# Two feed-forward stages behind a delta-rule attention: sorted rows scattered to DRAM, against rows kept in token order and gathered through a token list

## The chip, the cores and the metric

The kernel runs on one core of a Trainium2 chip. The metric is the time of the whole program on the device, in microseconds (us). Engines: TensorE (PE) multiplies matrices, VectorE (DVE), ScalarE (ACT) and GpSimd (POOL) work element by element, SyncE (SP) only issues transfers. ACT and POOL issue transfers too.

## What is computed

Four things follow one another; N = 3072 tokens (4 batches of 768), model width 384, hidden width 1024.

```python
for t in range(768):                       # delta-rule attention, 4 x 8 heads of width 48
    y[t] = q[t] @ state
    state += beta[t] * outer(k[t], v[t] - state.T @ k[t])      # k normalised
x = ((x @ w1) * (x @ w2)) @ w3 @ w_out     # dense part, for every token
e = argmax(x @ w_gate + bias[modality])    # one of 8 experts per token
gate = softmax(...)[e]
out[token] = gate * (relu(x @ w1[e]) @ w2[e])
```

The gate's weights are drawn large, so that the tokens fall on few experts: in the profiled execution three experts are loaded and 26 tiles of 128 tokens are computed.

## The kernel before

**First part, to about 652 us.** The tokens go in 24 units of 128 (6 groups of 4, one unit of each batch per group). Each engine has its own program, written out by hand turn by turn: in turn u, unit u is begun and unit u-1 ended, and six places `at` = 0..5 in a turn take one piece each of the dense part of an earlier group (`piece_of`: 24 pieces per group). The dense part of group c is: split of x into two roundings (`split_x`: ACT at L686 makes the upper one, DVE at L941 the rest), 16 products up (`up`, PE at L1427), 8 halves of products down (`down`, PE at L1445), which leave the 384 outputs and 8 logits of each row in `rows` (`take_row`, ACT at L703). `split_x(c)` stands in ACT's and DVE's programs one piece ahead of the group's first piece, behind the last `take_row` of the group before. ACT's `take_whole_t` (L642), which PE's `whole_x` (L1310) needs, stands ahead of that piece.

**Routing of a group**, one group later (DVE `choose`, `count`, `weigh`, `places`; PE `ranks`): the expert of each token, its gate, and its place, which is expert x 3200 plus its rank among the tokens of that expert. POOL's `scatter` (L563) then writes the four sets of 128 rows to `sorted_rows` in DRAM, each row to its place, with the token's number and gate in two more columns. ACT's `take_row` of the next group waits for that.

**Between the parts, about 669 to 712 us.** The last group is routed, PE counts the tokens of each expert, and DVE builds small tables by a chain of some 30 operations (L1120 to L1164): `fill_at`, where each expert's rows end; the order of the experts that have tokens (`ranks_ready`, at L1143); and for each tile its first row in `sorted_rows` and its expert (`table_ready`, at L1164). SP and ACT each write four blocks of 128 rows of padding behind the experts' rows (`fill_after`, L343 and L344), SP then loads the experts' weights (L492, 1.5 MB each for w1 and w2, with the first w2 held back until the first two x tiles have landed), ACT waits for all scatters and fills and loads the x tiles (`load_x`, L783 and L784). Weights are split like x (ACT L790, DVE L1180).

**Second part, the tiles.** The order on each engine for tile n is:

- PE: transposes of the hidden values of n (L1583), up product of n+1 (L1552), transposes of x of n+2 (L1532), down product of n (L1566).
- ACT: load of x of n+2, then the upper halves of the hidden values, perhaps half of a split of weights, hidden values and x of later tiles, the rest of the split.
- DVE: the same with the lower halves; last, when PE has ended the down product of n, `ys` = result x gate (L1215).
- POOL: waits for `ys` of n and writes it with an indirect DMA to the tokens' rows in `out` (L594). The token numbers are a column of the x tile. Padding rows have a number out of bounds and are left out.

The x buffers go round in four (`TURN`), so a load of x may be up to four tiles old. 24 tiles always run; further ones run under a condition (`tiles_that_may_be`), where POOL waits for each store to land (`stored_tile`).

Of the kernel before, what the change touches and what calls it, by code (L numbers as in the profile page):

```python
# [39 lines left out]
ROW = WX + 2  # L40
GATE, TOKEN = WX, WX + 1
CAP = N + P
# [18 lines left out]
def constants():  # L61
# [13 lines left out]
    token = ((u % B)[None, :] * S + (u // B)[None, :] * P + p[:, None]).astype(np.int32)  # L75
    fill = np.zeros((P, ROW), np.int32)
    fill[:, TOKEN] = NO_TOKEN
    small = np.concatenate([
        np.arange(E) - E,
        np.arange(E) * CAP,  # L80
        np.arange(N // P) * P,
        np.repeat(np.arange(TABLE), E),
        np.arange(TABLE) * P,
    ]).astype(np.float32)
    small = np.ascontiguousarray(np.broadcast_to(small, (P, small.size)))
    return {"planes": planes, "planes64": small_planes, "masks": masks, "token": token, "fill": fill, "small": small}
# [4 lines left out]
M_STARTS = M_PLACE + E  # L91
# [5 lines left out]
def program(nc, a, out):  # L97
    sorted_rows = nc.dram_tensor("sorted_rows", [(E + 1) * CAP, ROW], F32, kind="Internal").ap()
# [18 lines left out]
    with top:  # L117
# [9 lines left out]

        rows = sbuf(top, "rows", [P, B, ROW])
        rows_i = rows[:, :, :].bitcast(I32)
        token = sbuf(top, "token_sb", [P, UNITS], I32)  # L130
# [6 lines left out]
        place = sbuf(top, "place", [P, B], U32)  # L137
# [49 lines left out]
        hid = sbuf(late, "hid", [P, FF])  # L187
        raw = sbuf(late, "raw", [P, SLOTS * WE])
        xs = sbuf(late, "xs", [P, TURN, ROW])
        ys = sbuf(late, "ys", [P, TURN, DM])  # L190
        fill = sbuf(late, "fill_sb", [P, ROW], I32)
        fill_at = sbuf(late, "fill_at", [P, E], I32)
        ntile = sbuf(late, "ntile", [P, 4, E])
# [3 lines left out]
        table = sbuf(late, "table", [P, 4, TABLE + 1], I32)  # L197
        numbers = sbuf(late, "numbers", [P, M_END - M_STARTS])
# [7 lines left out]
        def plane64(k, n):  # L206
# [10 lines left out]
            hot_ready rank_done place_ready row_ready scattered dve_step count_done  # L217
            ranks_ready table_ready fill_ready filled expert_w1_in expert_w2_in upper_w1
            upper_w2 lower_w1 lower_w2 x_done xs_upper x_taken hid_done hid0_ready
# [119 lines left out]
        def fill_after(eng, experts_of):  # L339

            eng.wait_ge(q["fill_ready"], 1)
            for e in experts_of:
                row = eng.value_load(fill_at[0:1, e:e + 1], min_val=0, max_val=E * CAP - P)  # L343
                eng.dma_start(sorted_rows[bass.ds(row, P), :], fill[:, :].bitcast(F32)  # L344
                              ).then_inc(q["filled"], 16)
# [1300 lines left out]
```

## Time and profile before

| | before |
|---|---|
| median of 3 runs | 974.9 us (974.3 to 976.1) |
| the profiled execution: its own time | 973.82 us |
| its span, first to last instruction | 971.9 us |
| PE busy, matmul | 888.7 us (91%) |
| DVE / ACT / POOL busy | 490.3 / 343.2 / 274.4 us |
| mean granted TensorE clock | 0.965 of 2.4 GHz |

The profile is of one execution, and durations below come from it. Its time is 1.9 us more than its span, which lies around the instructions, and 1.1 us under the median of the three runs. A busy share is over the whole span, so it hides that the kernel has two dense parts with a gap between them.

### The profile page before, as it was taken

How to read it: one execution, taken by the hardware profiler on the slowest of the kernel's cores; microseconds unless marked ns; L12 is line 12 of the kernel's file. 1: busy time of each engine (PE TensorE's matmuls, PEld its weight loads, DVE VectorE, ACT ScalarE, POOL GpSimd, SP SyncE). 2: the span in 40 equal slices, each digit the busy share in tenths (PEclk: the TensorE clock that was granted, in tenths of full speed). 3: DMA queues.
4: the chain of work that ended last, by engine and by line, in shares of the span. 5: the costliest groups of instructions: out<-in, count | busy, mean ns of one | idle time of the engine just before them, and what ended most of it. 6: DMA issues, size and time to landing. Idle time of an engine off the chain costs nothing.

```text
span 971.9 us, 29550 instructions
## 1 busy us (share of the span) xinstructions
PE 888.7 (91%) x11972; PEld 741.6 (76%) x11973; DVE 490.3 (50%) x891; ACT 343.2 (35%) x628; POOL 274.4 (28%) x296
## 2 busy tenths in 40 slices
PE   5999989999999999899989999996379999999996
PEld 4766657788778877787778778785269899999985
DVE  2567666665755576557654752233265333333332
ACT  1344444444544453345424532220243222222221
POOL 5345544443454344434434210011000111101010
PEclk9999989999999999999989999998679999999998
DMA  7424311111121111111111010101931111111110
GB/s 247 129 84 140 84 38 37 38 38 38 37 72 38 38 38 54 54 38 38 44 52 33 17 45 10 33 33 56 326 143 43 42 42 41 39 46 44 41 41 21
DMA packets 46570, 60.13 MB, mean 62 GB/s; under 512 B 9192, under 2 KB 39160, under 8 KB 45552
## 3 DMA queue, kind: packets, MB, share of 16 engines
q1 hardware_dynamic: 38640, 42.35, 14.5%
q0 software_dynamic: 3200, 9.56, 2.6%
q10 hardware_dynamic: 4608, 6.46, 2.3%
q8 instruction: 93, 1.52, 0.6%
q14 instruction: 29, 0.24, 0.1%
HBM read 42.26 MB, written 11.77 MB: 56 GB/s over the span
## 4 chain that ended last, share of the span: by engine, by line
PE 80%; DVE 5%; POOL 5%; issue 3%; ACT 3%; another core or an unknown queue 1%; DMA 1%; SPq 1%; ACTq 0%; DVEq 0%; POOLq 0%
PE banks L1427 19%; PE banks L1552 12%; PE banks L1445 11%; PE banks L1566 11%; PE banks L1288 4%; PE banks L1397 3%; PE banks L1355 3%; PE banks L1583 2%; PE banks L1365 2%; PE banks L1248 2%; PE banks L1377 2%; POOL nm L543 1%; PE banks L1344 1%; POOL inv L547 1%
## 5 line engine op out<-in xcount | busy, mean ns | idle before, releaser
L1427 PE MATMUL banks<-xr,w12r 128*128 128x512 f32 x864 | 227.9, 412 | 7.6 <-DVE xr L941 7.5
L1427 PEld LDWEIGHTS banks<-xr,w12r 128*128 128x128 f32 x864 | 161.0, 194 | 45.5 <-issue 9.5
L1552 PE MATMUL banks<-experts,kept 128*128 x486 | 124.5, 411 | 11.0 <-DVE experts L1180 8.5
L1552 PEld LDWEIGHTS banks<-experts,kept 128*128 128x128 f32 x486 | 92.6, 195 | 32.4 <-issue 11.7
L1566 PE MATMUL banks<-experts,kept 128*128 x624 | 114.8, 340 | 0.0
L1445 PE MATMUL banks<-kept,hr 128*128 128x392 f32 x576 | 112.2, 347 | 0.0
L1566 PEld LDWEIGHTS banks<-experts,kept 128*128 128x128 f32 x624 | 107.1, 188 | 0.0
L1445 PEld LDWEIGHTS banks<-kept,hr 128*128 128x128 f32 x576 | 100.9, 188 | 2.0
L594 POOL DMA_INDIRECT out<-ys,xs x26 | 25.6, 984 | 259.7 <-DVE ys L1215 259.7
L531 POOL TENSOR_TENSOR kb<-keys,beta_sb 128x384 f32<-128x384 f32 x24 | 29.1, 1213 | 244.4 <-PE banks L1387 244.4
L874 DVE TENSOR_TENSOR picked<-inv,masks_sb 128x512 f16<-128x512 f16 x96 | 47.0, 489 | 77.0 <-ACT inv L630 76.0
L630 ACT ACTIVATE inv<-banks 128x512 f16<-128x512 f32 x96 | 57.2, 596 | 79.0 <-PE banks L1288 63.1
L636 ACT ACTIVATE inv<-banks 128x512 f16<-128x512 f32 x96 | 56.9, 593 | 51.0 <-PE banks L1291 45.0
L881 DVE STREAM_TRANSPOSE corr<-picked 128x512 f16<-128x512 f16 x96 | 68.3, 711 | 3.3
L828 ACT ACTIVATE kept<-banks 128x512 fp32r<-128x512 f32 x52 | 28.3, 596 | 104.4 <-PE banks L1583 104.4
L1288 PE MATMUL banks<-inv,corr 64*64 64x128 f16 x1152 | 47.5, 224 | 11.1 <-DVE corr L881 10.4
L563 POOL DMA_INDIRECT sorted_rows<-rows,place x24 | 23.4, 974 | 114.2 <-DVE place L1041 108.2
L947 DVE TENSOR_TENSOR asb<-asb,banks 128x512 f32<-128x512 f32 x48 | 32.9, 685 | 39.8 <-PE banks L1427 39.8
L1215 DVE TENSOR_SCALAR ys<-banks,xs 128x384 f32<-128x384 f32 x26 | 16.0, 617 | 71.4 <-PE banks L1566 71.4
L1397 PE MATMUL banks<-wo_x,w3T 128*128 128x392 f32 x128 | 51.5, 529 | 0.0
L1171 DVE TENSOR_SCALAR hid<-banks 128x512 f32<-128x512 f32 x27 | 18.6, 691 | 63.6 <-PE banks L1552 63.6
L804 ACT ACTIVATE hid<-banks 128x512 f32<-128x512 f32 x27 | 16.1, 598 | 92.5 <-PE banks L1552 92.5
(144 smaller groups left out, 1318.7 us busy)
## 6 DMA issues: line engine op xcount, KB each, us to landing
raw<-in_moe_w SPq DMA_DIRECT2D x6, 1536.0 KB, 7.3
kq<-in_qT SPq DMA_DIRECT2D x24, 256.0 KB, 2.7
xs<-sorted_rows ACTq DMA_DIRECT2D x28, 197.0 KB, 2.4
kraw<-in_k SPq DMA_DIRECT2D x24, 192.0 KB, 2.4
vals<-in_v SPq DMA_DIRECT2D x48, 96.0 KB, 2.5
w3T<-in_w3T SPq DMA_DIRECT2D x8, 512.0 KB, 4.3
w<-in_w SPq DMA_DIRECT2D x8, 384.0 KB, 4.2
xT<-yT SPq DMA_DIRECT2D x48, 64.0 KB, 2.1
```

The source lines that it names most:

```text
L630: nc.scalar.activation(inv[:, u % 2, 1].rearrange("p (k g) t -> p k (g t)", k=2), all_pairs(1), ACT.Copy).then_inc(right_taken[level], 1)
L636: nc.scalar.activation(inv[:, u % 2, 0].rearrange("p (k g) t -> p k (g t)", k=2), all_pairs(0), ACT.Copy).then_inc(x_taken[level], 1)
L874: nc.vector.tensor_tensor(picked[:], inv[:, u % 2, 1], masks[:, level - 1:level, :].to_broadcast([P, H, R]), ALU.mult).then_inc(masked[lev ...
L881: nc.vector.transpose(corr[:, u % 2, level % 2].rearrange("p g t -> p (g t)"), picked[:].rearrange("p g t -> p (g t)")).then_inc(part_read ...
L947: nc.vector.tensor_tensor(asb[:, j % 2], asb[:, j % 2], psum[:, UP + 1, :], ALU.mult).then_inc(q["h_made"], 1)
L1288: last = mm(pairs_of(g)[rows_of(x)], part, inv[rows_of(x), u % 2, :, g, :], start=True, stop=True)
L1355: last = mm(told_of(o)[rows_of(x), j, :], xfin[rows_of(x), u % 2, o * HH + j, :], rest[rows_of(x), o * HH + j, :], start=True, stop=True)
L1397: last = mm(psum[:, UP + i % 2, 0:WX], w3T[:, i % W_SLOTS, k, :], wo_x[:, k, :], start=(k == 0), stop=(k == FT - 1))
L1427: last = mm(psum[:, UP + w, :], w12r[:, p, w, k, j * P:(j + 1) * P], xr[:, r, k, :], start=(k == 0 and p == r), stop=(k == KT - 1 and p == 1))
L1445: last = mm(psum[:, UP + t % 2, 0:WX], hr[:, p, j, t * P:(t + 1) * P], w34r[:, r, j, :], start=(j == 0 and p == r), stop=(j == FT - 1 and ...
L1552: last = mm(psum[:, f, :], xsr[:, w, p, k, :], experts[:, bass.ds(slot * (2 * WE) + at, FF // 2)], start=(k == 0 and p == r), stop=(k == K ...
L1566: last = mm(psum[:, 4 + w, 0:DM], hTr[:, p, k, :], experts[:, bass.ds(slot * (2 * WE) + at, DM)], start=(k == 0 and p == r), stop=(k == FT ...
```

## The change

Rows go to DRAM in token order, by plain transfers on SP's queue. The row has 385 columns: the gate takes the place of the first logit. POOL's scatters, the padding rows and the fills on SP and ACT are gone. `place` is now expert x 3072 plus rank, taken apart into a lane (0..127) and a column (0..191). In the gap of buffers after the attention, POOL builds for each unit one-hot matrices of lanes, times a token number (`list_lane`, 128 columns), and of columns (`list_column`, 192 columns), in f16; for the last group DVE builds the lanes. PE multiplies them, 24 products summed in one bank, which gives for each expert tile a column of token numbers. DVE makes two indices of them by five operations: one to gather with, one to store with. In the tile loop ACT loads nothing; POOL reads the tile's column number, copies the column of indices to `index_now` and gathers x of n+2 by an indirect DMA, then waits for `ys` of n and stores it, as before. ACT's `split_x` of the groups 1 to 5 stands two pieces ahead of the group instead of one. The wait for the first two x tiles moves from the first expert's w2 to the second expert's w1.

```diff
@@ SP
+                        keep_rows(piece[0] - 1)
+            def keep_rows(c):
+                sp.wait_ge(q["row_ready"], c + 1)
+                sp.dma_start(kept_rows.rearrange("(b c p) n -> c p b n", b=B, c=C)[c], rows[:, :, 0:ROW]
+                             ).then_inc(q["rows_kept"], 16)
-            fill_after(sp, range(0, E, 2))
-                        if k == 0 and name == "w2":
+                        if k == 1 and name == "w1":
                             for w in range(2):
                                 sp.wait_ge(x_in[w], 16)
@@ POOL
-            def scatter(c):
-                for t in range(B):
-                    nc.gpsimd.indirect_dma_start(
-                        sorted_rows[:, :], bass.IndirectOffsetOnAxis(ap=place[:, t:t + 1], axis=0),
-                        rows[:, t, :], None).then_inc(q["scattered"], 16)
+            def list_lane(t):
+                nc.gpsimd.tensor_scalar(lane_is[:, t, :], small[:, M_LANE:M_LANE + P], lane[:, t:t + 1],
+                                        token[:, t:t + 1], ALU.is_equal, ALU.mult
+                                        ).then_inc(q["lane_listed"], 1)
+            def list_column(t):
+                nc.gpsimd.tensor_scalar(column_is[:, t, :], slots[:], column[:, t:t + 1], None, ALU.is_equal
+                                        ).then_inc(q["column_listed"], 1)
+            def gather(n, r):
+                at = pool.value_load(table[0:1, 0, bass.ds(n, 1)], min_val=0, max_val=NO_SLOT)
+                nc.gpsimd.tensor_copy(index_now[:, r, :], index[:, bass.ds(at, 1), :].rearrange("p o k -> p (o k)")
+                                      ).then_inc(q["index_taken"], 1)
+                pool.wait_ge(q["index_taken"], n + 1)
+                alone(pool)
+                nc.gpsimd.indirect_dma_start(
+                    xs[:, r, :], None, kept_rows[:, :],
+                    bass.IndirectOffsetOnAxis(ap=index_now[:, r, 0:1], axis=0)).then_inc(x_in[r], 16)
+            pool.wait_ge(q["table_ready"], 1)
+            pool.wait_ge(q["index_ready"], 1)
+            pool.wait_ge(q["rows_kept"], 16 * C)
+            gather(0, 0)
+            gather(1, 1)
             def tile(i, r):
-                pool.wait_ge(q["ys_ready"], i * TURN + r + 1)
+                n = i * TURN + r
+                ahead = (r + 2) % TURN
+                since(pool, stored[ahead], 16 * (i + (r + 2) // TURN))
+                gather(n + 2, ahead)
+                pool.wait_ge(q["ys_ready"], n + 1)
                 alone(pool)
                 nc.gpsimd.indirect_dma_start(
-                    out[:, :], bass.IndirectOffsetOnAxis(
-                        ap=xs[:, r, TOKEN:TOKEN + 1].bitcast(U32), axis=0),
+                    out[:, :], bass.IndirectOffsetOnAxis(ap=index_now[:, r, 1:2], axis=0),
                     ys[:, r, :], None, bounds_check=N - 1, oob_is_err=False).then_inc(stored[r], 16)
@@ ACT
-                for c in group_begun(u, at, 1):
-                    split_x(c)
+                for ahead in (1, 2):
+                    for c in group_begun(u, at, ahead):
+                        if (c > 0) == (ahead == 2):
+                            split_x(c)
-            fill_after(act, range(1, E, 2))
-                since(act, stored[ahead], 16 * (i + (r + 2) // TURN))
-                load_x(n + 2, ahead)
@@ DVE
+                link(v.tensor_reduce(place[:, now], key, AX.X, ALU.add))
+                link(v.tensor_scalar(column[:, now], place[:, now], 0.5 - P / 2, ROUNDS_TO_P, ALU.add, ALU.add))
+                link(v.tensor_scalar(column[:, now], column[:, now], -ROUNDS_TO_P, None, ALU.add))
+                v.tensor_tensor(lane[:, now], place[:, now], column[:, now], ALU.subtract
+            for t in range(UNITS - B, UNITS):
+                v.tensor_scalar(lane_is[:, t, :], small[:, M_LANE:M_LANE + P], lane[:, t:t + 1],
+                                token[:, t:t + 1], ALU.is_equal, ALU.mult).then_inc(q["last_lane_listed"], 1)
+            dve.wait_ge(q["slots_found"], 1)
+            link(v.tensor_scalar(late_at[:], numbered, 0.0, float(N + 1), ALU.is_lt, ALU.mult))
+            link(v.tensor_tensor(found[:], numbered, late_at[:], ALU.add))
+            v.tensor_scalar(index[:, 0:NO_SLOT, 0], found[:], -1.0, 0.0, ALU.add, ALU.max)
+            link(v.tensor_scalar(late_at[:], found[:], 0.0, float(NO_TOKEN), ALU.is_equal, ALU.mult))
+            v.scalar_tensor_tensor(index[:, 0:NO_SLOT, 1], found[:], -1.0, late_at[:], ALU.add, ALU.add
+                                   ).then_inc(q["index_ready"], 1)
@@ PE
+                    last = mm(psum[:, 5, 0:NO_SLOT], lane_is[:, t, :], column_is[:, t, :],
+                              start=(t == 0), stop=(t == UNITS - 1))
+            place_tokens(range(UNITS - B))
             ranks(C - 1)
             mm(psum[:, 6, 0:E], planes[:, C_ONE, :], seen[:], start=True, stop=True
                ).then_inc(q["count_done"], 1)
+            place_tokens(range(UNITS - B, UNITS)).then_inc(q["slots_found"], 1)
```

## Rows read from the trace of the kernel before

**Rows 1.** Page, part 4: share of the chain that ended last, by engine.
```profile
PE 80%; DVE 5%; POOL 5%; issue 3%; ACT 3%; another core or an unknown queue 1%; DMA 1%; SPq 1%; ACTq 0%; DVEq 0%; POOLq 0%
```
**Rows 2.** Stretches: length, busy of PE, PEld, DVE, ACT, POOL, clock, DMA, GB/s.
```profile
672.00:691.00 19.00, 1.66 (x7) 1.60 (x8) 8.35 (x43) 0.62 (x1) 3.84 (x4) 0.50 0.74 232
...
724.00:940.00 216.00, 216.00 (x1193) 195.25 (x1192) 80.08 (x119) 52.81 (x95) 22.64 (x23) 1.00 0.12 41
```
**Rows 3.** Chain of work at the first tiles: start, us, what.
```profile
728.01 0.33 PE banks L1532 x3
728.34 4.17 PE banks L1566 x24
```
**Rows 4.** Chain, one tile in the middle.
```profile
742.08 0.87 PE banks L1583 x8
...
747.18 0.33 PE banks L1532 x3
```
**Rows 5.** Timeline of that tile: start, length, what, idle before.
```profile
742.12 0.62 DVE L1215 TENSOR_SCALAR ys<-banks,xs 128x384 f32<-128x384 f32 x1 [2.93 <-PE banks L1566]
...
743.62 0.98 POOL L594 DMA_INDIRECT out<-ys,xs  x1 [5.69 <-DVE ys L1215]
```
**Rows 6.** POOL's prices: transfer to landing; value load (ns); gap between scatters; two operations.
```profile
out<-ys,xs POOLq DMA_INDIRECT x26, 2.5
...
L334 POOLq TENSOR_LOAD <-table x1: 502/502/502, 947.6 to 947.6; - x1
...
POOL sorted_rows L563 <- issue: 5.1, 18, 0.3
...
L543 POOL TENSOR_TENSOR nm<-am,planes_sb 128x256 f16<-128x256 f32 x48 | 37.0, 770 | 12.8 <-DVE am L865 12.8
...
L583 POOL MEMSET keys<- 128x128 f32 x1 | 0.2, 204 | 0.3 <-POOLq L1638 0.3
```
**Rows 7.** L784, the 28 loads of x tiles: issue to landing.
```profile
DMA to landing us min/median/max: 2.1/2.4/8.6
```
**Rows 8.** Timeline of the first tiles, where ACT and DVE also split weights.
```profile
725.83 0.61 DVE L1215 TENSOR_SCALAR ys<-banks,xs 128x384 f32<-128x384 f32 x1
...
728.95 2.77 ACT L790 ACTIVATE experts<-raw  x1
...
732.16 3.36 DVE L1180 TENSOR_TENSOR experts<-raw,experts  x1
```
**Rows 9.** Timeline between the parts.
```profile
672.29 0.64 PE L1455 MATMUL banks<-hot,planes_sb 128*128 128x32 f32 x2 [3.04 <-DVE seen L1018]
...
674.14 0.36 DVE L1120 TENSOR_TENSOR over<-banks,numbers 128x192 f32<-128x192 f32 x1
...
675.71 5.01 SPq L344 DMA_DIRECT2D sorted_rows<-fill_sb  x4
...
677.63 0.17 DVE L1143 CAST table<-ttab 128x8 int32<-128x8 f32 x1
...
681.72 0.24 DVE L1164 TENSOR_SCALAR table<-ttab 128x33 int32<-128x33 f32 x1
```
**Rows 10.** Chain between the parts.
```profile
682.87 7.24 DMA raw<-in_moe_w
...
694.90 6.54 PE banks L1552 x18
```
**Rows 11.** Timeline at a boundary of groups; last, that wait over all groups (total, times, longest).
```profile
231.75 0.60 ACT L642 ACTIVATE inv<-banks 128x512 f16<-128x512 f32 x1 [0.37 <-PE banks L1301]
...
233.98 0.44 PE L1310 MATMUL banks<-inv,corr 64*64 64x64 f16 x16
...
234.48 1.66 ACT L686 ACTIVATE xr<-xT 128x512 fp32r<-128x512 f32 x3
...
236.82 2.29 PE L1427 MATMUL banks<-xr,w12r 128*128 128x512 f32 x9 [1.45 <-DVE xr L941]
...
PE banks L1427 <- DVE xr L941: 7.5, 6, 1.9
```

More of the change, by code:

```diff
@@ L39 @@
 E_SCALE = 1024.0
-ROW = WX + 2
-GATE, TOKEN = WX, WX + 1
-CAP = N + P
+GATE = DM
+ROW = DM + 1
+CAP = N
+HI = CAP // P
+NO_SLOT = E * HI
+ROUNDS_TO_P = float(3 * P << 22)
 TILES = N // P + E - 1
@@ L136, in program @@
         lred = sbuf(top, "lred", [P, 5, B])
[L137 removed]
+        place = sbuf(top, "place", [P, UNITS])
+        lane = sbuf(top, "lane", [P, UNITS])
+        column = sbuf(top, "column", [P, UNITS])
         work = ExitStack()
@@ L438, in turn @@
                     send(u - 2)
+                for at in range(SPLITS):
+                    piece = piece_of(u, at)
+                    if piece and piece[0] and piece[1] == WEIGH:
+                        keep_rows(piece[0] - 1)
[3 more added lines that the diff above has]
+                             ).then_inc(q["rows_kept"], 16)
             load_k(0)
@@ L464, in _ @@
             sp.wait_ge(q["y_taken"], UNITS + 1)
-            sp.dma_start(fill[:], a["fill"]).then_inc(q["b_in"], 16)
+            sp.dma_start(slots[:], a["slots"]).then_inc(q["slots_in"], 16)
             sp.dma_start(numbers[:], a["small"][:, M_STARTS:]).then_inc(q["b_in"], 16)
-            sp.wait_ge(q["b_in"], 80)
-            sp.dma_start(sorted_rows[E * CAP:E * CAP + P, :], fill[:, :].bitcast(F32)
-                         ).then_inc(q["filled"], 16)
-            fill_after(sp, range(0, E, 2))
+            for u in range(UNITS + 2, last_turn() + 1):
+                for at in range(SPLITS):
+                    piece = piece_of(u, at)
+                    if piece and piece[0] and piece[1] == WEIGH:
+                        keep_rows(piece[0] - 1)
+            keep_rows(C - 1)
             sp.wait_ge(q["ranks_ready"], 1)
@@ L573, in turn @@
                     beta_mask(u + 1)
-                for at in range(SPLITS):
-                    piece = piece_of(u - 1, at)
-                    if piece and piece[0] and piece[1] == RANK:
-                        scatter(piece[0] - 1)
                 if live(u + 1):
@@ L585, in _ @@
             pool.wait_ge(q["const_in"], 64)
-            for u in range(-2, last_turn() + 1):
+            for u in range(-2, UNITS + 1):
                 turn(u)
-            scatter(C - 1)
-            def tile(i, r):
-                pool.wait_ge(q["ys_ready"], i * TURN + r + 1)
+            pool.wait_ge(q["y_taken"], UNITS + 1)
+            for b in range(B):
+                pool.wait_ge(sent[b], 64 * C)
+            nc.gpsimd.memset(index[:, NO_SLOT, 0:1], 0)
+            nc.gpsimd.memset(index[:, NO_SLOT, 1:2], NO_TOKEN).then_inc(q["no_slot_set"], 1)
@@ new lines, in _ @@
+            pool.wait_ge(q["b_in"], 64)
+            pool.wait_ge(q["slots_in"], 16)
+            for c in range(C):
+                pool.wait_ge(q["place_ready"], c + 1)
+                for t in range(c * B, c * B + B):
+                    if c < C - 1:
+                        list_lane(t)
+                    list_column(t)
+            def gather(n, r):
[3 more added lines that the diff above has]
+                pool.wait_ge(q["index_taken"], n + 1)
```

101 lines of the change are left out of this document (52 added, 49 removed).

## The prediction

> **What bounds the kernel now.** I read the chain of waits first: PE holds 80% of it [rows 1]. Then the stretches: from 724 to 940 us PE is busy all the time at the full clock, and from 672 to 691 us it does almost nothing, at half clock [rows 2]. So there are two dense parts, where whatever delays PE lengthens the run, and a gap between them, set by a chain through DVE, SP's transfers and ACT. The timeline then shows, in each part, what stands closest to PE's path. The change touches three places: group boundaries in the first part, the gap, and every tile of the second. I take the tiles first, because 25 of them multiply whatever one costs.
>
> **Tiles: where the new load of x stands.** In a tile of the middle PE ends a down product at 742.08, transposes and does the up product, and wants x of the tile after next at 747.18, 5.10 us later [rows 4]. Today ACT asks for that x well ahead, so nobody waits. After the change POOL asks for it, and POOL is in order: the gather for tile n+2 stands behind the store of tile n-1, which stands behind `ys` of n-1, which stands behind PE's down product of n-1. The four buffers don't help, since the request itself is late. The path from there, step by step:
> - `ys` runs 742.12 to 742.74, and the store on POOL 743.62 to 744.60 [rows 5]: both stay.
> - The value load takes 0.50 us on POOL [rows 6], with register work some 0.75 (estimate). It may run under the store (0) or after it (0.75). The sequencer should be free while the engine writes descriptors, so I take 0.2.
> - The copy of 128x2 numbers: POOL's 128x128 memset takes 0.20 [rows 6], so 0 to 0.2; I take 0.1.
> - The gather waits for that copy by semaphore, like the store for `ys`: the store starts 0.88 after `ys` ends [rows 5]. Back to back, without a wait, the gap is 0.3 [rows 6]. I take 0.88, because the wait is there; 0.3 is the low end.
> - Landing: 2.5 us from the start for the indirect store [rows 6], 2.1 at the least for plain loads of x [rows 7]. An indirect load is not in the trace; I take 2.5, ends 2.1 and 2.6.
>
> So x lands at 744.60 + 0.2 + 0.1 + 0.88 + 2.5 = 748.28, which is **1.1 us after PE wants it**, and 5.54 after `ys` ends. The low ends give 747.0, just in time (0); the high ones 749.03 (1.9). The wait can't be made up: PE's down product is behind the transposes of x, `ys` behind that, and the next gather behind `ys`. The loop becomes a ring of DVE, POOL, DMA and PE, and each tile pays.
>
> 26 stores mean 26 tiles [rows 6], and gathers 0 to 27. The first three are asked ahead of any store, so 25 can be late. Four of them are special:
> - x 3: DVE does `ys` of tile 0 late, behind a split of weights, ending 726.44 [rows 8]. x lands at 731.98; PE wants it at 728.01 [rows 3]: 4.0.
> - x 4: ACT's split started 0.94 after the transposes of x 3 and takes 2.77, DVE's then 3.36, `ys` 0.61 [rows 3, 8]. From 731.98 that is 739.7, and x 4 lands at 745.2. PE wants it 0.33 + 4.17 + 5.10 after 731.98, at 741.6: 3.7.
> - x 26: the loop has ended, POOL waits for the last store to land (0.88 + 2.5 after `ys`), does two value loads (1.5), copy, start and landing (3.48): 8.4 against 4.44, so 3.9.
> - x 27: the same with one value load: 3.2.
>
> Sum: 14.8 for the four, and 21 x 1.1 = 23.1 for the others: **+37.9**. With the low ends the four give 10.5 and the others 0; with the high ones 18 and 40.
>
> **Group boundaries.** PE waits 7.5 us in six places for the split of x [rows 11], and at the one shown ACT begins it at 234.48, behind the last `take_row`. One piece earlier it goes ahead of L642 at 231.75 and takes 1.66, so L642 ends at some 234.0 and PE's L1310, which needs it, is at 233.98: no loss beyond 0.1. DVE has the operands 2.7 us earlier, more than the 1.45 that PE waited. The first group keeps its place. 5/6 of 7.5: **-6.2**; ends 0 (if the y values have not landed by then, ACT holds up everything behind) and -7.5.
>
> **Removed from the first part.** POOL's scatters and two small DVE operations per group cost nothing today: POOL sits idle before the keys of each turn, and no chain went through them. SP's `keep_rows` waits for the gates, which are made earlier in the same turn than the y values SP has just waited for: nothing queued behind it is late. If it were, the loads of k and q two turns ahead would cover it. The one-hots of the first 20 units are made by POOL after 615 us, 40 operations of 0.2 to 0.77 us each [rows 6], at most 31 us, before 669. PE's 20 products fit in the 3.04 us in which it waited before 672.29 [rows 9] if each takes up to 0.15 us. If not, each tenth of a microsecond more is 2 us. I count 0.
>
> **The gap.** DVE gains two small operations in `places`, four one-hots (0.25 each, between small operations and the 0.36 of 128x192 [rows 9]) and loses one: +1.3, so the tables are ready at 681.96 + 1.3 = 683.3 [rows 9]. Five operations of 0.4 for the indices follow: 685.3. Then value load, copy and start (0.75 + 0.1 + 0.88): the first gather begins at 687.0. SP loses the fills, which kept it until 680.72 [rows 9]; it then needed 2.15 us to send w1 [rows 10]. Now it starts when the order of the experts is there, at 677.8 + 1.3 = 679.1 [rows 9], w1 goes at 681.3 and lands at 688.5, 1.6 sooner. But w2 of the same expert now goes right behind it, 1.5 MB more, and until some 695 the gather shares the DMA engines with it. Loads of x took 2.4 in the median and 8.6 at most, the latter with weights in flight [rows 7]. Alone the first x lands at 689.5, and then w1 sets the start: 1.6 gained. With 8.6 it lands at 695.6; transposes, ACT and DVE (some 1.8) put the first up product at 697.4 against 694.90 [rows 10], 2.5 lost. I take nearly that end, **+2.0**, since the weights are in flight the whole time.
>
> The Trainium skill (DMA: Bandwidth & Descriptors, Queues, rings and completion order) says that each DMA engine takes turns between queues packet by packet, with some 9 to 17 descriptors in a typical packet. The 8 rows that an engine has of a gather would then be one packet, and pass after one packet of weights; by this the gap would gain the 1.6 and the sum would be 3.6 lower. The 8.6 us row speaks against it.
>
> **Sum.** +37.9 - 6.2 + 2.0 = +33.7 on the profiled 973.8, so 1007.5, and the median lies 1.1 above: **1008.6 us**.
>
> **Rivals.**
> 1. *The gather just makes it* (chance 0.08). With all low ends the steady wait is 0; the four special ones (10.5), the boundaries (-7.5) and the gap (-1.6) leave +1.4: 976. For it: each low end is in a row. Against it: all four have to hold together, and the semaphore latency of 0.88 is seen at each store.
> 2. *Faster* (0.07). Besides rival 1, w2's early arrival lets DVE do `ys` of tiles 0 and 1 without a split of 3.36 us ahead of it, and the special waits shrink from 10.5 to about 4: 4 - 7.5 - 1.6 = -5, 970. It decides at a path from `ys` to landed x of 4.44 us; I get 5.54.
> 3. *The clock falls* (0.05). If gaps in every tile make the chip grant half the clock, as it does in the idle stretch [rows 2], an up product takes 6.54 instead of 4.2 us [rows 10], and a tile some 5 us more: +125, 1130. Against it: the first part has a wait of 1.45 us [rows 11] and runs on.
> The forecast has 0.80. Its own ends are +15 (steady wait 0.5) and +60 (1.9, and nothing gained at the boundaries): 990 to 1035. The range, 980 to 1038, also takes in part of rival 1. About 0.2% is what a measurement of this kernel can tell from no change; that bound and the cases give faster 0.08, same 0.03, slower 0.89.
>
> **What would show it.** Right: PE's L1532 twin waits for the DMA of x about 1.1 us in each of some 21 tiles, and 3 to 4 us in four; a period of some 10.7 us instead of 9.6 (5.10 + 0.33 + 4.17); POOL's idle time before its store shrinks to about 5 us. The waits of L1427 on L941 all but vanish. The first gather takes more than 6 us to land. Wrong: if POOL's gather starts less than 1 us after the store ends, or an indirect load lands in 2 us or less, the steady wait goes and rival 1 or 2 holds; if the gather starts over 2 us behind the store, the time is above 1030.

## The result and the profile after

On the same chip the changed kernel takes 1034.5 us in the median of 4 runs (1031.6 to 1042.7), the kernel before 975.4: ratio 1.062, 95% interval [1.056, 1.068], so **59 us slower**. The forecast was 1008.6 in a range of 980 to 1038.

| | before | after |
|---|---|---|
| the profiled execution: its own time | 973.82 us | 1035.74 us |
| its span | 971.9 us | 1033.9 us |
| PE busy, matmul | 888.7 us (91%) | 911.2 us (88%) |
| DVE / ACT / POOL busy | 490.3 / 343.2 / 274.4 us | 503.3 / 346.0 / 328.4 us |
| mean granted TensorE clock | 0.965 | 0.951 |

The page after, its first part and the chain that ended last. Where nothing but PE held a large share before [rows 1], the transfer of `xs` has 8% of the chain now:

```profile
PE 911.2 (88%) x11996; PEld 756.5 (73%) x11997; DVE 503.3 (49%) x905; ACT 346.0 (33%) x628; POOL 328.4 (32%) x375
...
PE 66%; DMA 9%; issue 8%; DVE 8%; POOL 5%; ACT 2%; POOLq 2%; DVEq 0%; SPq 0%; ACTq 0%
PE banks L1482 19%; PE banks L1637 12%; PE banks L1500 10%; DMA xs<-kept_rows,index_now 8%; PE banks L1343 4%; PE banks L1410 3%; PE banks L1452 2%; PE banks L1303 2%; PE banks L1420 2%; PE banks L1432 2%; DVE ys L1270 2%; PE banks L1603 2%; PE banks L1623 1%; PE banks L1399 1%; DVE xr L981 1%
```

The timeline of one tile in the middle, the twin of [rows 4, 5] (start, length, what, and in brackets the idle time before and what ended it):

```profile
802.33 0.62 DVE L1270 TENSOR_SCALAR ys<-banks,xs 128x384 f32<-128x384 f32 x1 [3.52 <-PE banks L1637]
...
802.72 4.44 PE L1623 MATMUL banks<-experts,kept 128*128 x18
...
803.87 1.02 POOL L645 DMA_INDIRECT out<-ys,index_now  x1 [8.89 <-DVE ys L1270]
804.86 0.23 POOL L621 COPY index_now<-index 128x2 uint32 x1
805.89 0.99 POOL L626 DMA_INDIRECT xs<-kept_rows,index_now  x1 [0.80 <-POOL index_now L621]
...
809.01 0.55 PE L1603 MATMUL banks<-planes_sb,xs 128*128 128x128 f32 x3 [1.85 <-DMA xs<-kept_rows,index_now]
...
809.50 6.01 PE L1637 MATMUL banks<-experts,kept 128*128 x24
```

The ring of the prediction is there: `ys`, store, copy, gather, landing, PE. PE has ended its up product at 807.16 and stands until 809.01. Two things are not as predicted. The gather takes 3.12 us from its start to PE's first transpose (I took 2.5). And the 24 products of the down product behind the wait take 6.01 us, where 13 of the 21 tiles from 3 to 23 show 4.5 in the same view. In the 6 us before PE's transposes the granted clock is 1.00, in the 6 us behind them 0.72, between its two levels, so a part of this product ran at half the clock (length; busy of PE, PEld, DVE, ACT, POOL; clock, DMA, GB/s). The third line has the whole stretch from 724 to 990 us, where before the clock was 1.00 and PE was never idle [rows 2]:

```profile
803.00:809.00 6.00, 4.16 (x18) 3.00 (x16) 1.98 (x3) 1.68 (x3) 2.22 (x3) 1.00 0.20 66
809.00:815.00 6.00, 5.99 (x26) 5.83 (x27) 0.56 (x1) 0.49 (x1) 0.00 (x0) 0.72 0.00 0
...
724.00:990.00 266.00, 228.55 (x1139) 200.61 (x1139) 66.89 (x107) 45.84 (x85) 46.54 (x63) 0.94 0.10 31
```

Of the waits of that stretch (total, times, longest) PE's for x is the one that is new:

```profile
PE banks L1603 <- DMA xs<-kept_rows,index_now: 37.5, 21, 2.2
```

The view of the tile `xs` gives the time from a gather's issue to its landing. The 7.4 is the third gather, issued at 667.37 us beside the experts' weights; nothing waited for it.

```profile
DMA to landing us min/median/max: 3.0/3.2/7.4
```

**Where the time went.** With the starts of `ys` as milestones (tile 0 at 725.83 before and 699.87 after, tile 2 at 742.12 and 730.11, tile 23 at 943.44 and 989.94, tile 25 at 962.61 and 1024.19), the two spans compare like this:

| stretch | before | after | change | predicted |
|---|---|---|---|---|
| start to tables ready | 681.96 | 658.28 | -23.7 | -4.9 |
| tables to the first up product | 12.94 | 10.70 | -2.2 | +0.7 |
| to `ys` of tile 0 | 30.93 | 30.89 | 0 | 0 |
| tiles 1 and 2 | 16.29 | 30.24 | +13.9 | +7.7 |
| tiles 3 to 23 | 201.32 | 259.83 | +58.5 | +23.1 |
| tiles 24 and 25 | 19.17 | 34.25 | +15.1 | +7.1 |
| to the end | 9.29 | 9.71 | +0.4 | 0 |
| sum | | | +62.0 | +33.7 |

The direction is right, and every large term is too small: the tiles lost more than twice what I gave them, and the first part gained 19 us that I did not see at all. These two are what the experiments are about.

### The profile page after: what moved, and what is told of

Same layout as the page of the kernel before. It is cut to its first block, busy times and chain, and to the rows that moved or that the text cites. A ratio compares the mean times of both kernels' runs of the same rounds, so it can differ in the third digit from the quotient of the medians.

```text
span 1033.9 us, 29628 instructions
## 1 busy us (share of the span) xinstructions
PE 911.2 (88%) x11996; PEld 756.5 (73%) x11997; DVE 503.3 (49%) x905; ACT 346.0 (33%) x628; POOL 328.4 (32%) x375
## 4 chain that ended last, share of the span: by engine, by line
PE 66%; DMA 9%; issue 8%; DVE 8%; POOL 5%; ACT 2%; POOLq 2%; DVEq 0%; SPq 0%; ACTq 0%
PE banks L1482 19%; PE banks L1637 12%; PE banks L1500 10%; DMA xs<-kept_rows,index_now 8%; PE banks L1343 4%; PE banks L1410 3%; PE banks L1452 2%; PE banks L1303 2%; PE banks L1420 2%; PE banks L1432 2%; DVE ys L1270 2%; PE banks L1603 2%; PE banks L1623 1%; PE banks L1399 1%; DVE xr L981 1%
## 5 line engine op out<-in xcount | busy, mean ns | idle before, releaser
L1482 PE MATMUL banks<-xr,w12r 128*128 128x512 f32 x864 | 222.4, 404 | 0.7 <-DVE xr L981 0.7
L1482 PEld LDWEIGHTS banks<-xr,w12r 128*128 128x128 f32 x864 | 156.8, 189 | 36.3 <-DVE xr L981 1.1
L1637 PE MATMUL banks<-experts,kept 128*128 x624 | 135.9, 381 | 0.0
L1623 PE MATMUL banks<-experts,kept 128*128 x486 | 124.2, 410 | 8.5 <-DVE experts L1235 8.1
L1637 PEld LDWEIGHTS banks<-experts,kept 128*128 128x128 f32 x624 | 127.9, 219 | 2.9 <-issue 0.7
L1623 PEld LDWEIGHTS banks<-experts,kept 128*128 128x128 f32 x486 | 92.8, 196 | 29.4 <-issue 9.2
L645 POOL DMA_INDIRECT out<-ys,index_now x26 | 26.5, 1020 | 274.9 <-DVE ys L1270 274.9
L1603 PE MATMUL banks<-planes_sb,xs 128*128 128x128 f32 x84 | 17.4, 322 | 71.1 <-DMA xs<-kept_rows,index_now 71.0
L1603 PEld LDWEIGHTS banks<-planes_sb,xs 128*128 128x128 f32 x84 | 9.9, 156 | 82.9 <-DMA xs<-kept_rows,index_now 68.8
```

What stands on the lines that cost most here:

```text
L1482: last = mm(psum[:, UP + w, :], w12r[:, p, w, k, j * P:(j + 1) * P], xr[:, r, k, :], start=(k == 0 and p == r), stop=(k == KT - 1 and p == 1))
L1603: last = nc.tensor.transpose(psum[:, 6 + r % 2, k * P:(k + 1) * P], xs[:, r, k * P:(k + 1) * P], ident)
L1623: last = mm(psum[:, f, :], xsr[:, w, p, k, :], experts[:, bass.ds(slot * (2 * WE) + at, FF // 2)], start=(k == 0 and p == r), stop=(k == K ...
L1637: last = mm(psum[:, 4 + w, 0:DM], hTr[:, p, k, :], experts[:, bass.ds(slot * (2 * WE) + at, DM)], start=(k == 0 and p == r), stop=(k == FT ...
```

## The experiments

Twelve kernels ran, four to a chip. The kernel before does not take the same time on every chip: 956.2 us on chip 6 (e1 to e4), 974.6 on chip 1 (e5 to e8), 974.0 on chip 8 (e9 to e12). So ratios are against the kernel before on the same chip, and the difference itself became a question (e3, e11, e12). The profiled execution of the kernel before belongs with the 974s.

### e1: the gathers asked for one tile earlier

```diff
+            gather(2, 2)
...
-                ahead = (r + 2) % TURN
-                since(pool, stored[ahead], 16 * (i + (r + 2) // TURN))
-                gather(n + 2, ahead)
+                ahead = (r + 3) % TURN
+                since(pool, stored[ahead], 16 * (i + (r + 3) // TURN))
+                gather(n + 3, ahead)
```

> The changed kernel with one edit: POOL gathers x of tile n+3 instead of n+2, into the buffer of tile n-1, once that tile's store has landed. Theory A (the tiles lose because the request for x is late, and the falling clock is only a consequence of PE's waits): POOL asks some 5.3 us after ys, x lands some 8.5 us after ys, PE wants it 14 us after ys, so no wait; the period goes back to 9.6 us, the clock to 1.00, the tile part from 348 to 260 us from the second up product on: time about 947 us, 28 below the kernel before. Rival B (software gathers on POOL slow PE or the transfers whatever their place): waits of 1 us or more per tile stay, time above 975.

Measured: 948.4 us, 0.9914 [0.9895, 0.9933] of the kernel before. The stretch of the tiles:

```profile
724.00:910.00 186.00, 186.00 (x1029) 169.00 (x1029) 61.43 (x98) 40.36 (x78) 42.59 (x58) 1.00 0.13 40
```

PE is busy all the time at the full clock, and `ys` comes every 9.4 to 9.8 us, as before. Tiles 3 to 23 take 201.81 us (201.32 before), and the four special tiles lose no more than 0.2 us. The ring was the whole loss in the tiles. The gather itself is no faster (3.2 us in the median); it is only behind a store one tile older. On this chip this kernel is 0.9% faster than the kernel before.

### e2: the index taken a tile ahead, the gather in its old place

```diff
+            def take_index(n, r):
                 at = pool.value_load(table[0:1, 0, bass.ds(n, 1)], min_val=0, max_val=NO_SLOT)
                 nc.gpsimd.tensor_copy(index_now[:, r, :], ...
                                      ).then_inc(q["index_taken"], 1)
+            def gather(n, r):
...
-                since(pool, stored[ahead], 16 * (i + (r + 2) // TURN))
                 gather(n + 2, ahead)
+                after = (r + 3) % TURN
+                since(pool, stored[after], 16 * (i + (r + 3) // TURN))
+                take_index(n + 3, after)
```

> The changed kernel with one edit: the value load and the copy of the index column for tile n+3 stand ahead of the wait for ys, so that only store and gather stand behind it; the gather stays where it was. Theory A (the steps I listed, in series): the copy (0.23 us) and the part of the 0.80 us start that a wait costs (0.5, since starts back to back are 0.30 apart) leave the ring; the full-clock period goes from 11.7 to 11.0 us, time about 1034 - 25 x 0.7 = 1017, less if the clock holds more often. Rival (the start of an indirect DMA costs 0.8 us by itself whatever precedes it): 0.23 only, about 1028.

Measured: 1004.1 us, 1.0499 [1.0475, 1.0523]. Its timeline at a store, a gather and the transposes that wait for it:

```profile
805.15 1.02 POOL L652 DMA_INDIRECT out<-ys,index_now  x1 [7.30 <-DVE ys L1277]
806.47 1.00 POOL L628 DMA_INDIRECT xs<-kept_rows,index_now  x1 [0.31 <-issue]
...
809.76 0.55 PE L1610 MATMUL banks<-planes_sb,xs 128*128 128x128 f32 x3 [1.14 <-DMA xs<-kept_rows,index_now]
```

The gather follows the store by 0.31 us in place of 1.00, and PE's wait drops from 1.85 to 1.14: the same 0.7 us. Tiles 3 to 23 take 233.6 us (11.1 each). The clock in its tiles is 1.00, with a wait of 1.1 in each tile. So the copy and the semaphore behind it are 0.7 us of the ring. The expectation had 1017 us for these 0.7 in 25 tiles; the time is 13 us below it, and it had allowed for that where the clock holds, as it does here. Of what is left of the ring, the landing is the largest step.

### e3: the scatters put back beside e1

Four groups' rows are written by index where POOL had its scatters; they go to rows of DRAM that nobody reads.

```diff
+            def spare(c):
+                pool.wait_ge(q["place_ready"], c + 1)
+                pool.wait_ge(q["row_ready"], c + 1)
+                alone(pool)
+                for t in range(B):
+                    nc.gpsimd.indirect_dma_start(
+                        spare_rows[:, :], bass.IndirectOffsetOnAxis(ap=spot[:, t:t + 1], axis=0),
+                        rows[:, t, 0:ROW], None).then_inc(q["spared"], 16)
...
+                    since(act, q["spared"], 16 * B * min(c, 4))
...
+                link(v.tensor_copy(spot[:], place[:, now]))
```

The last two lines are ACT's wait for the writes ahead of its next rows, and a small copy on DVE that makes the index.

> e1 with POOL's indirect writes of the rows put back at their old place in POOL's turns for groups 0 to 3, to a tensor nobody reads (plain transfers on SP stay too). Theory C (the first part gained 24 us mostly because these writes are gone: they hold up ACT, DVE and PE for 4 us each time): the tables are ready 16 to 20 us later than in e1, time e1 + 18, ACT waits of 4.3 us from a releaser that the profile can't name come back. Rival D (the gain came from the earlier split of x and from the granted clock): e1 + 1 or less.

Measured: 949.7 us, 0.9926 [0.9905, 0.9947], 1.35 above e1, where the runs of each spread over 1.2 and 2.2 us. The expected 18 us are not there. Nor is the 1.35 in the first part: the last `ys` begins at 936.55 us (936.48 in e1), and the difference is behind it, 11.1 us to the end against 9.8. e11 and e12 have the same longer end, for which no trace shows a reason. On this chip the scatters are nearly free.

### e4: e1 with the split of x back in its place

```diff
-                for ahead in (1, 2):
-                    for c in group_begun(u, at, ahead):
-                        if (c > 0) == (ahead == 2):
-                            split_x(c)
+                for c in group_begun(u, at, 1):
+                    split_x(c)
```

> e1 with ACT's split of x put back to one piece ahead of its group. Theory C: PE waits for the split again, 1.5 to 1.9 us at five boundaries: e1 + 6. Rival D: e1 + 20 or more.

Measured: 955.0 us, 0.9987 [0.9976, 0.9999], **6.6 above e1**. PE's waits in the first part (total, times, longest), e4:

```profile
PE banks L1481 <- DVE xr L980: 7.5, 6, 2.0
```

and the same line in e1:

```profile
PE banks L1483 <- DVE xr L982: 0.5, 1, 0.5
```

The wait of [rows 11] is back, 7.5 in six places, and costs nearly what it says. The term of -6.2 was right. On chip 6, e1 + 6.6 (split) + 1.35 (scatters) = 956.3, and the kernel before takes 956.2 there. That the sum fits so closely is in part luck: the 1.35 is at the end of the program, the kernel before was not traced on this chip, and the rest of the change (lists, tables, gap) is not in the sum.

### e5 and e6: both kernels once more, on another chip

> The kernel before, unchanged, for a profile beside the others. In e1 to e4 it took 956.2 us where the first measurement had 975.4, and e3 showed the scatters at 1.3 us. Theory F (the 4.3 us stalls of all engines in the turns with scatters belong to the place where the program runs, and not to the scatters alone): the profile of a run of 956 us has the scatters at the same places and no such stall, its tables are ready at 663 us instead of 682, and the tile part is 260 us as before. Rival G (the tile part or the gap is what differs): the 19 us are found behind 669 us.

> The changed kernel, unchanged, beside e5, e7 and e8. Theory F: it has no scatters in the first part, so it takes the same 1032 to 1040 us here, and the change costs some 78 us instead of 59 where the kernel before takes 956. Rival G: it gains 19 us as well, 1015.

Neither has an edit. e5 (the kernel before): 974.9 us, 0.9997 [0.9986, 1.0009], the same; one of its ten runs took 1697.6, for which no trace shows a reason. e6 (the changed kernel): 1038.9 us, 1.0649 [1.0627, 1.0671]. A trace of the kernel before at 956 us, which would show what it takes 18 us more for on this chip, is missing. e5's waits from 250 to 640 us have a candidate (total, times, longest):

```profile
ACT inv L630 <- remote: 12.8, 3, 4.3
...
DVE corr L893 <- remote: 9.3, 3, 3.3
...
ACT inv L636 <- remote: 6.7, 1, 6.7
```

"remote" is a wait that no instruction of the profile ends. The waits of ACT and DVE run in part at the same time, so their sum is not the loss. The profile of before had them too: its page shows "another core or an unknown queue 1%" [rows 1]. e6 has none.

### e7: the changed kernel with PE kept busy in the wait

```diff
+                for _ in range(16):
+                    nc.tensor.transpose(psum[:, 6 + r % 2, 384:512], ident, ident)
```

The 16 transposes of a unit matrix stand between the up product and the transposes of x; nothing reads them.

> The changed kernel with one edit: in every tile PE does 16 transposes of the identity (0.11 us each) into free columns between the up product and the transposes of x, where it waits. Theory H (down products of 5.9 us are ones at half the clock, and the clock falls because PE waits some 2 us in each tile): PE has hardly any gap, the clock is 1.00 in the tile part, every down product takes 4.2 to 4.4 us, the period is 11.7 us in all tiles: 1.6 us less in some 9 tiles, about 1020. Rival (the slow down products come from something else, the gather's traffic for one): they stay at 5.9 us, 1034 or more.

Measured: 1022.5 us, 1.049 [1.0464, 1.0516]: **16.4 below e6, with more work**. The stretch in e6:

```profile
724.00:990.00 266.00, 228.41 (x1115) 200.75 (x1114) 66.09 (x106) 45.69 (x84) 46.66 (x63) 0.92 0.10 31
```

and in e7:

```profile
724.00:990.00 266.00, 258.20 (x1520) 230.94 (x1521) 69.44 (x110) 47.87 (x88) 48.86 (x66) 1.00 0.11 33
```

The clock is 1.00 in place of 0.92. The timeline of e7 shows a tile in which the ring is untouched and only the gap is filled:

```profile
800.08 0.62 DVE L1270 TENSOR_SCALAR ys<-banks,xs 128x384 f32<-128x384 f32 x1 [3.51 <-PE banks L1637]
...
804.74 1.91 PE L1659 MATMUL banks<-planes_sb 128*128 128x128 f32 x16
...
806.68 0.55 PE L1603 MATMUL banks<-planes_sb,xs 128*128 128x128 f32 x3
807.14 4.50 PE L1637 MATMUL banks<-experts,kept 128*128 x24
...
811.67 0.62 DVE L1270 TENSOR_SCALAR ys<-banks,xs 128x384 f32<-128x384 f32 x1 [3.33 <-PE banks L1637]
```

x still arrives 6.60 us after `ys` begins, and the down product takes 4.5. Tiles 3 to 23 take 247.3 us, against 264.2 in e6 and 201.3 before. That separates the two parts of e6's loss there: 46.0 from the ring at the full clock (2.2 a tile) and 16.9 from the clock. Eleven of e6's 21 down products there take 5.9 to 6.0 us, 1.5 more than the others, which is the same 16.9 within 0.4. The filling does not help the last two tiles, whose waits are longer (34.7 us against 33.4).

### e8: a plain read in the gather's place

The choice of rows is left out: each tile reads the first 128 rows in DRAM.

```diff
-                nc.gpsimd.indirect_dma_start(
-                    xs[:, r, :], None, kept_rows[:, :],
-                    bass.IndirectOffsetOnAxis(ap=index_now[:, r, 0:1], axis=0)).then_inc(x_in[r], 16)
+                pool.dma_start(xs[:, r, :], kept_rows[0:P, :]).then_inc(x_in[r], 16)
```

> The changed kernel with POOL's gather replaced by a plain read, from POOL's queue too, of the same 128 rows of 385 numbers each time: it leaves out the choice of rows, so the outputs are of other tokens. Theory I (an indirect load takes 3.1 us to land where plain ones take 2.4 because of the rows' own addresses): landing 2.4 to 2.6, period 11.1, waits 0.6 us shorter in 25 tiles, time 1018 or, if the clock holds, 1005. Rival (a load on POOL's queue takes 3.1 us whatever it reads): the same time as e6.

Measured: 1004.8 us, 1.0303 [1.0285, 1.0322], 34 below e6. The view of `xs` in e8:

```profile
DMA to landing us min/median/max: 2.6/2.7/4.7
```

and one of its reads in the timeline:

```profile
810.62 0.56 POOL L626 DMA_DIRECT2D xs<-kept_rows  x1 [0.60 <-POOL index_now L621]
```

The plain read starts 0.60 after the copy (0.80) and lands in 2.7 us (3.2): 0.7 us less per tile, and with that the clock mostly holds (0.99 from 724 to 960). It is e2's saving by another way, and e2's time within 0.7 us, though on another chip.

### e9: the second weight matrix held back again, beside e1

```diff
-                        if k == 1 and name == "w1":
+                        if k == 0 and name == "w2":
```

> e10 with SP's wait for the first two row tiles put ahead of the first expert's second weight matrix, as the kernel before had it (it now stands ahead of the second expert's first matrix). Theory, that the second matrix's transfer is what makes the first gather land 4.6 us after its start in the changed kernel, where those in the loop take 3.1: the first gather lands about 1.5 us sooner, the first up product begins 1 to 1.5 us sooner, and the time is 1 to 1.5 us under e10's unless the second matrix's own split then comes late. Rival, that a first gather is slow for another cause, or that the chain into the first up product runs through other work: no change within 0.5 us, or slower by up to 2 us for the later matrix.

Measured: 948.3 us, 0.9727 [0.9702, 0.9753]; e10, its reference, 947.5. No gain. The first gather and the first transposes in e9:

```profile
662.53 1.19 POOL L626 DMA_INDIRECT xs<-kept_rows,index_now  x1 [0.92 <-POOL index_now L621]
...
666.49 0.87 PE L1604 MATMUL banks<-planes_sb,xs 128*128 128x128 f32 x3 [12.97 <-DMA xs<-kept_rows,index_now]
```

That is 3.96 us, against 4.62 in e10 (661.61 to 666.23). So the second matrix in flight costs the first gather 0.7 us, not 1.5. From the start of the last operation on the tables (658.53 and 657.62) the first up product comes 0.4 us sooner, and the second one 0.4 later (27.4 us against 27.0). The move of that wait is worth nothing either way.

### e10, e11, e12: e1, scatters and plain writes on a chip where the kernel before takes 974

> e1 once more, as the reference for this batch: the list order with gathers issued three tiles ahead. Both theories expect what e1 gave in its own time, 947 to 950 us, on whatever chip this is, if the changed order is as insensitive to the chip in its first part as the runs so far say (the kernel before took 956 us on one chip and 975 on another); if the chip itself were slower for every kernel, it would take about 2% more where the kernel before takes 975.

e10: 947.5 us, 0.9723 [0.9697, 0.9749]. The order without scatters takes the same on chips 6 and 8 (948.4 and 947.5).

> e10 with indirect writes of the first four groups' rows put back where the kernel before had its scatters (they go to rows that nobody reads). On the first chip these cost 1.35 us (e3 against e1), and the kernel before took 956 us there. Theory, that the scatters are what stalls the engines by some 4 us in each of four turns on the chips where the kernel before takes 975: if this chip is such a one, e10 plus 15 to 20 us, with ScalarE waits of about 4 us in the turns that hold the writes; if it is one where the kernel before takes 956, e10 plus 1 to 2 us again. Rival, that those stalls have another cause in the kernel before (its fills, its order of loads): e10 plus 1 to 2 us on either chip.

e11 has e3's edit, line for line: 966.3 us, 0.9909 [0.9882, 0.9936]. **The same writes that cost 1.35 us on chip 6 cost 18.8 here.** In the profiled executions, 18.4 us apart, 17.1 are there by the last `ys` and 1.3 lie in the longer end. Its waits that nothing in the profile ends, from 250 to 640 us:

```profile
ACT inv L696 <- remote: 12.2, 3, 4.3
DVE corr L950 <- remote: 6.6, 2, 3.3
ACT inv L702 <- remote: 5.9, 1, 5.9
```

They are e5's, at the same two operations of ACT and one of DVE, and of nearly the same lengths; ACT has one of 3.6 to 5.9 us in each of the four turns that hold the writes. The timeline of e11 at one of the four groups:

```profile
285.22 1.15 POOL L580 DMA_INDIRECT spare_rows<-rows,spot  x1 [0.17 <-issue]
...
286.68 0.97 POOL L580 DMA_INDIRECT spare_rows<-rows,spot  x1 [0.30 <-issue]
...
287.95 0.96 POOL L580 DMA_INDIRECT spare_rows<-rows,spot  x1 [0.30 <-issue]
...
289.22 0.96 POOL L580 DMA_INDIRECT spare_rows<-rows,spot  x1 [0.30 <-issue]
290.21 0.60 ACT L696 ACTIVATE inv<-banks 128x512 f16<-128x512 f32 x1 [3.63 <-remote]
```

and of e3, the same instructions on chip 6:

```profile
285.25 1.15 POOL L580 DMA_INDIRECT spare_rows<-rows,spot  x1 [0.17 <-issue]
...
286.71 0.97 POOL L580 DMA_INDIRECT spare_rows<-rows,spot  x1 [0.31 <-issue]
...
287.11 0.60 ACT L696 ACTIVATE inv<-banks 128x512 f16<-128x512 f32 x1 [0.48 <-PE banks L1361]
```

The first three of POOL's four writes start at the same times to 0.03 us, the fourth at 289.22 and 289.30. ACT's operation after L1361 runs at 287.11 on the one chip and at 290.21 on the other. From 284 to 296 us PE is busy 9.59 us in e11 and 11.93 in e3. Of the 18.4 us by which e11's span exceeds e10's, 15.8 lie before the tables (ready at 673.7 and 657.9). With e4's split, which delays the tables by 7.3 (665.4 against 658.1 in e1), that is 23.1 of the 23.7 us by which the change brought them forward.

> e11 with plain writes of the same rows and size on GpSimd's queue in place of the indirect ones. If it is the writes' indirectness that stalls the engines (where e11 shows it), this takes e10's time plus 0 to 2 us; if it is any write on GpSimd's software queue during the turns, it takes e11's time. Where e11 itself costs only 1 to 2 us, both say e10 plus 0 to 2 us and the run decides nothing.

```diff
-                    nc.gpsimd.indirect_dma_start(
-                        spare_rows[:, :], bass.IndirectOffsetOnAxis(ap=spot[:, t:t + 1], axis=0),
-                        rows[:, t, 0:ROW], None).then_inc(q["spared"], 16)
+                    pool.dma_start(spare_rows[(c * B + t) * P:(c * B + t + 1) * P, :], rows[:, t, 0:ROW]
+                                   ).then_inc(q["spared"], 16)
```

e12: 949.3 us, 0.9742 [0.9716, 0.9768], 1.8 above e10, with no wait on "remote"; its last `ys` begins 0.9 us before e10's, and only the longer end is left. Plain writes of the same bytes on the same queue stall nothing, and neither do the copy on DVE and ACT's wait, which e12 keeps. So in these runs it takes two things together: writes by index, and such a chip. Two points are not separated. Each chip was used on one occasion only, so the chip and the occasion are not told apart. And e12 changes where the rows land (next to one another, in place of by their place) together with the way in which they are addressed.

## Why the prediction was right or wrong

**The tiles: right in mechanism, mis-sized by half.** The ring from `ys` through store and gather to PE is what the change costs, in each tile, and e1 takes the whole of it away by moving nothing but the request (and so the copy of its index). From the end of `ys` at 802.95 to PE's start at 809.01 it takes 6.06 us; I had 5.54. Step by step against the prediction's path: store 0.92 + 1.02 (0.88 + 0.98), value load 0, since it runs under the store (0.2), copy 0.2 (0.1), start of the gather 0.80 (0.88), landing 3.12 (2.5). **The step that failed is "An indirect load is not in the trace; I take 2.5, ends 2.1 and 2.6"**: an indirect load takes 3.0 at the least, beyond the high end. I had bounded a gather by a scatter, and it is slower than both the scatter (2.6) and the plain read on the same queue (2.7, e8). PE's wait was then 1.8 in the mean (37.5 over 21), not 1.1: 0.5 of the difference is the longer ring, and 0.2 is that PE wants x already 4.83 us after `ys` begins (807.16), not 5.06.

The Trainium skill (DMA: Bandwidth & Descriptors, Anatomy of one DMA, SWDGE path) gives some 2.0 us plus the bytes at 436 GB/s for a transfer from POOL's queue, which would be 2.5 us for the 197 KB of a tile (an estimate from that page). e8's plain read comes near it with 2.7; the page does not set a gather apart, and the runs show 3.1 to 3.2 for one.

At the full clock a tile costs 2.2 us more (e7), of which 1.8 is the wait. The other 0.4 lies behind it: from PE's first transpose of x to the next `ys` there are 4.99 us in e7 (806.68 to 811.67), where PE does not even stand before it, and 4.53 before (747.18 to 751.71). What makes these 0.4 was not tried alone. I had counted the wait alone.

**The clock: rival 3, in part.** I gave it 0.05 and 125 us. It is neither absent nor complete. Behind the wait some down products run in part at half the clock (6.0 us for 4.5), and others run at the full clock. In the profiled execution of after 8 of the 21 down products of tiles 3 to 23 are slow, in e6 11 of 21. The length of the one wait does not decide it: one of 1.68 us stands before a slow product (871.30 us) and one of 1.94 before a fast one (911.35). e7 prices it at 16.9 us for e6; for the profiled execution of after, 12.5 are left of the 58.5 us when the ring's 46.0 are taken off. The argument against it, "the first part has a wait of 1.45 us and runs on" [rows 11], compared one wait every 100 us with one in each tile of 12. The Trainium skill (TensorE: Matmul & The Clock Gate, HAM oscillation) describes loops in which a wait for a DMA in every turn sends the clock down again and again; the runs agree in kind, with the granted clock at 0.94 and 0.92 here, and 1.00 where the wait is 1.1 us (e2) or filled (e7).

**The four special tiles: 29.0, predicted 14.8.** The waits are 6.1, 3.3, 5.5 and 5.0 us (4.0, 3.7, 3.9 and 3.2). They add up to 19.9. One reason that the waits are longer than forecast: the gathers of x 3, 26 and 27 take 3.9 us to land, more than the 3.2 of the median. The other 9 us of the 29.0 were not tried alone, but the down products behind these four waits take 5.6, 6.8, 6.2 and 6.3 us in place of some 4.5, with a granted clock of 0.63 to 0.77, which is 7 of the 9.

**Group boundaries: right.** -6.2 predicted, 6.6 measured (e4), and the waits of L1427's twin fell from 7.5 us to 0.7.

**"Removed from the first part. POOL's scatters ... cost nothing today": wrong on such a chip**, by some 16 us up to the tables (e11; nothing on chip 6 that shows there), and it is the largest thing that the change gains. "No chain went through them" was true of POOL's idle time and of the semaphores. But the waits on "remote" stood in the trace of before, 13 us of them at ACT's L630 alone, in turns in which POOL scatters, and [rows 1] had a share that belonged to no engine. I read past it as noise. A wait that no instruction ends is a reason to look at what else happens at that time.

**The gap: -2.2 from the tables to the first up product, predicted +0.7.** Gather begins 3.76 us after the tables (3.7 predicted), but the first x is there 4.6 us later and not 8.6, nor the "more than 6" of the signs: "I take nearly that end" was the wrong end, by 4 us. The 8.6 in [rows 7] is the load of the third tile, issued at 702.28. The first two loads, at 687.55, also had a weight matrix in flight (it landed at 690.1 [rows 10]) and took 2.8 to 3.1 us; they were the rows for this place. After the change the order is the same: the first gather takes 4.5 us and the second 3.4, and the third, beside the next matrices, 7.4. So weights in flight do hold a gather up, by more or less, but PE waits only for the first; with the second matrix held back that one still takes 4.0 (e9). The Trainium skill's rule on turns packet by packet (DMA: Bandwidth & Descriptors, Queues, rings and completion order) gave 3.6 less for the sum than I took. For the first gather the trace agrees with it better than with my choice; the 7.4 of the third speaks against so small a delay. The list's products and one-hots cost nothing that shows in the first part: PE's 20 products take 1.82 us at 643.90, ahead of the ranks, and the last four wait 4.3 us for POOL, inside the time from the last group to the tables that was there before.

**Why the number came out in the range all the same.** The tiles were 50 us short (87.5 against 37.9), the gain ahead of them 22 us short (25.9 against 4.2), and the two errors have opposite signs. That is luck: the clock and the scatters have nothing to do with each other. On chip 1 the same kernel took 1038.9 us (e6), 0.9 above the range. On chip 6 the kernel before takes 956. The changed kernel was not run there, but its order without scatters did not differ between chips (e1, e10), so it should be some 80 us slower there, where I forecast 34. That is an estimate.

## What to carry to other kernels

When a load moves to a queue in which stores wait for results, it becomes as late as the last store ahead of it, however many buffers there are: ask for it one tile further ahead, and the cost is gone (e1: 948 us against 1035 to 1039). Count in a wait that comes in every turn of a PE loop also what the clock does with it, and try filling the wait. And where a profile shows waits that nothing in it ends, look for what coincides with them; here it was worth some 17 us, on the chips that show them.

## What the runs showed of the hardware that was not expected

- **Indirect writes stall other engines on some chips and not on others.** With four scatters of 128 rows in a group, ACT and DVE stand 2.7 to 6.7 us without a releaser on chips 1 and 8, and not at all on chip 6 (e5, e11 against e3). That is 18.8 us for 16 scatters on chip 8 and 1.35 on chip 6. Plain writes of the same rows cost 1.8 on chip 8 (e12). Some 1.3 us of each of the three is a longer end of the program. The 28 gathers and 26 indirect stores of the tiles do not slow e1 on chip 8: it takes 948.4 and 947.5 us on the two. What differs between the chips (or the occasions, one to a chip), and why these writes stall and the later ones do not, stays open.
- **A gather lands in 3.0 us at the least and 3.2 in the median**, a plain read of as many bytes on the same queue in 2.6 and 2.7, an indirect store in 2.6. Beside weight matrices in flight a gather took up to 7.4 (after) and 8.2 (e9). On POOL, a DMA behind a semaphore of POOL's own copy starts 0.80 us after it when indirect and 0.60 when plain; without that wait 0.31 (e2).
- **Useless products made the kernel 16 us faster** (e7): 16 transposes in each tile hold the granted clock at 1.00, where it was 0.92 with waits of 1.8 us in tiles of 12. With waits of 1.1 us it was 1.00 without them (e2).
